# Rows of the sixth slot on turned by DMA instead of TensorE, in a routed expert kernel on one core

## The reference

```python
e_idx = np.argmax(x @ w_gate, axis=1)
...
for e in range(E):                       # E = 8, F = 1024, D = 512
    mask = e_idx == e
    h = np.maximum(x[mask] @ w1[e], 0.0)
    ye = h @ w2[e]
    out[mask] = gate_w[mask, None] * eom[mask, e, None] * ye
```

## Time and profile before

| | |
|---|---|
| median of 3 runs | 860.55 us (859.25 to 861.95) |
| the profiled execution | 863.49 us |
| its span in the trace | 861.7 us |
| TensorE busy | 827.6 us, 96% of the span |
| VectorE, ScalarE, GpSimd busy | 572.5, 383.6, 180.2 us |
| mean granted TensorE clock | 0.995 of full speed |

### The profile page before, as it was taken

One profiled execution on the slowest core, in us unless ns is written; L12 is line 12 of the kernel. 1 busy time (PEld: TensorE's weight loads), 2 busy tenths in 40 slices (PEclk: granted clock), 3 DMA queues, 4 the chain that ended last, 5 costly groups with the idle time before them and its releaser, 6 DMA issues.

```text
span 861.7 us, 19310 instructions
## 1 busy us (share of the span) xinstructions
PE 827.6 (96%) x7018; PEld 549.2 (64%) x7019; DVE 572.5 (66%) x1200; ACT 383.6 (45%) x798; POOL 180.2 (21%) x208
## 2 busy tenths in 40 slices
PE   7999999999999999999999999999899999999995
PEld 5888777876555555555455555556577767777773
DVE  4778788877887998998898898855532444222221
ACT  5766667776555555555555555523111111111110
POOL 4444376663000001001001001010121222111100
PEclk9999999999999999999999999999999999999998
DMA  7255565541483884875784875485253852656610
GB/s 223 98 178 180 166 205 181 177 136 61 172 286 132 267 257 173 267 258 172 256 256 183 256 256 183 162 300 193 92 182 139 313 197 76 238 201 219 233 70 14
DMA packets 76554, 163.83 MB, mean 190 GB/s; under 512 B 39574, under 2 KB 43926, under 8 KB 69840
## 3 DMA queue, kind: packets, MB, share of 16 engines
q1 hardware_dynamic: 70576, 146.20, 50.3%
q0 software_dynamic: 5760, 16.80, 5.7%
q10 hardware_dynamic: 160, 0.07, 0.0%
HBM read 109.44 MB, written 47.47 MB: 182 GB/s over the span
## 4 chain that ended last, share of the span: by engine, by line
PE 70%; DVE 12%; issue 6%; DMA 5%; ACT 3%; POOL 2%; another core or an unknown queue 1%; DVEq 0%; POOLq 0%; ACTq 0%; SPq 0%
PE ps L876 18%; PE ps L865 15%; PE ps L971 11%; PE ps L959 11%; DMA arena<-split 4%; PE ps L781 4%; PE ps L726 3%; PE ps L753 3%; ACT arena L1073 2%; DVE arena L1256 2%; DVE arena L1510 2%; POOL arena L555 1%; PE ps L740 1%; DVE yrow L1475 1%; DVE relu L1566 1%
## 5 line engine op out<-in xcount | busy, mean ns | idle before, releaser
L865 PE MATMUL ps<-arena,w_in_sb 128*128 128x384 f16 x1152 | 200.9, 326 | 0.0
L876 PE MATMUL ps<-w_out_sb,arena 128*128 128x512 f16 x576 | 171.2, 379 | 5.0 <-DVE stage L1571 4.9
L865 PEld LDWEIGHTS ps<-arena,w_in_sb 128*128 128x128 f16 x1152 | 112.3, 98 | 80.9
L959 PE MATMUL ps<-x_sb,arena 128*128 128x128 f16 x2112 | 121.7, 219 | 3.9 <-DMA arena<-split 3.0
L959 PEld LDWEIGHTS ps<-x_sb,arena 128*128 128x128 f16 x2112 | 119.3, 98 | 8.1 <-issue 4.9
L1233 ACT ACTIVATE x_sb<-ps 128x512 f16<-128x512 f32 x54 | 31.6, 596 | 206.7 <-PE ps L959 172.4
L971 PE MATMUL ps<-arena,x_sb 128*128 128x512 f16 x528 | 119.7, 383 | 2.2 <-DVE x_sb L1667 2.2
L876 PE MATMUL ps<-w_out_sb,stage 128*128 128x512 f16 x288 | 109.1, 379 | 0.0
L1073 ACT ACTIVATE arena<-ps,arena 128x128 f32<-128x128 f32 x288 | 79.4, 382 | 55.4 <-DVE arena L1258 51.2
L1205 ACT ACTIVATE arena<-relu 128x384 f16<-128x384 f32 x96 | 50.0, 521 | 109.5 <-DVE relu L1566 108.3
L876 PEld LDWEIGHTS ps<-w_out_sb,arena 128*128 128x128 f16 x576 | 55.8, 98 | 65.4 <-issue 7.2
(11 more groups left out here) (210 smaller groups left out, 976.9 us busy)
## 6 DMA issues: line engine op xcount, KB each, us to landing
arena<-split SPq DMA_DIRECT2D x36, 1024.0 KB
arena<-in_moe_w SPq DMA_DIRECT2D x16, 2048.0 KB
split<-arena SPq DMA_DIRECT2D x16, 2048.0 KB, 7.5
arena<-in_qkt SPq DMA_DIRECT2D x15, 576.0 KB, 6.2
stage<-in_moe_w_in SPq DMA_DIRECT2D x16, 512.0 KB, 4.1
stage<-in_moe_w_out SPq DMA_DIRECT2D x16, 512.0 KB, 5.3
x_sb<-rows POOLq DMA_DIRECT2D x27, 257.0 KB
arena<-in_v SPq DMA_DIRECT2D x32, 128.0 KB, 4.4
```

Source lines behind the costliest of these rows:

```text
L865: last = nc.tensor.matmul(ps[:, HB[f % GB], 0:BN], w_in_sb[:, lw, c, f * P:(f + 1) * P], xt[:, a, lx, c, :], start=c == 0 and lw + lx == 0 ...
L876: last = nc.tensor.matmul(ps[:, YB + r, :], g_sb[lg_][:, f % GB, r * P:(r + 1) * P], w_out_sb[:, lw, f, :], start=f == 0 and lg_ + lw == 0 ...
L959: last = nc.tensor.matmul(ps[:, bank, f % 4 * P:(f % 4 + 1) * P], w1_sb[b][:, lw, c, f * P:(f + 1) * P], xgt[:, a, lx, c, :], start=c == 0 ...
```

## The change

Rows of slots 0 to 4 are turned on TensorE as before. From slot 5 (`TURN_AT`) on, ScalarE issues one DMA transpose for a slot: it reads the slot's rows from `xg` and writes them turned into a new buffer `turned`; VectorE copies that into `xgt` in place of the PSUM bank. There are four row buffers (`XB4`) and four turned buffers. ScalarE issues the DMA for slot s + 4 right after the relus of slot s, and waits for the rows' load before it. GpSimd loads slot s + 5 right after it has stored slot s. The loops over slots of ScalarE, VectorE and GpSimd are written out; TensorE keeps its loop, without the transposes.

```diff
+XB4, TURN_AT = 4, 5
...
-        xg = spare[:, 0:2 * XW].rearrange("p (a d) -> p a d", a=2)
+        xg = spare[:, 0:XB4 * XW].rearrange("p (a d) -> p a d", a=XB4)
+        turned = spare[:, 14336:14336 + XB4 * 2 * DM].rearrange("p (a k n) -> p a k n", a=XB4, k=2 * DC)
...
@@ GpSimd
-            def next_load(s, a):
-                row = slot_start(s)
-                pool.wait_ge(xg_read, s - 1)
+            def load(s, row=None):
+                row = slot_start(s) if row is None else row
+                if s >= XB4:
+                    pool.wait_ge(xg_read, s - XB4 + 1)
                 carry()
-                load(row, a)
+                pool.dma_start(xg_words[:, s % XB4, :], rows[bass.ds(row, P), :]).then_inc(xg_loaded[s % XB4], 16)
...
-            for s in range(EARLY, EARLY + 2):
-                load(starts[s - EARLY], s % 2)
+            for s in range(EARLY, EARLY + 4):
+                load(s, starts[s - EARLY])
             store(1, 1, True)
-            for s in range(EARLY + 2, EARLY + 4):
-                next_load(s, s % 2)
-            store(2, 0, True)
-            next_load(7, 1)
-            store(3, 1, True)
-            with pool.Fori(0, (SLOTS - 9) // 2) as i:
-                for a in range(2):
-                    next_load(i * 2 + (a + 8), a)
-                    store(i * 2 + (a + 4), a)
-            next_load(SLOTS - 1, 0)
-            for s in range(SLOTS - 5, SLOTS):
-                store(s, s % 2)
+            for s in range(2, SLOTS):
+                store(s, s % 2, s < 4)
+                if s + 5 < SLOTS:
+                    load(s + 5)
@@ TensorE
             def used_slot(s, a, need, b):
                 slot_hidden(a, b)
-                if more:
-                    slot_transposes(s + 2, a, turn)
                 pe.wait_ge(ew2_loaded, need)
                 pe.wait_ge(og_ready, s - 1)
                 slot_output(s, a, b)
@@ ScalarE
+            def turn_rows(s):
+                a = s % XB4
+                act.wait_ge(xg_loaded[a], s // XB4 * 16 + 16)
+                if s >= TURN_AT + XB4:
+                    act.wait_ge(xgt_ready, s - XB4 + 1)
+                act.dma_start_transpose(turned[:, a], xg[:, a, 0:2 * DM]).then_inc(turned_rows[a], 16)
             relu_slot(1, 1)
             relu_slot(2, 0)
-            with act.Fori(0, (SLOTS - 3) // 2) as i:
-                relu_slot(i * 2 + 3, 1)
-                relu_slot(i * 2 + 4, 0)
+            for s in range(TURN_AT, TURN_AT + 2):
+                turn_rows(s)
+            for s in range(EARLY, SLOTS):
+                relu_slot(s, s % 2)
+                if s + 4 < SLOTS:
+                    turn_rows(s + 4)
@@ VectorE
             def slot_in(s, a, bank=None):
-                dve.wait_ge(xg_transposed, s + 1)
+                if s < TURN_AT:
+                    dve.wait_ge(xg_transposed, s + 1)
+                    src = ps[:, a if bank is None else bank, :].bitcast(F16)
+                else:
+                    dve.wait_ge(turned_rows[s % XB4], (s - TURN_AT) // XB4 * 16 + 16)
+                    src = turned[:, s % XB4].rearrange("p k n -> p (k n)")
```

More of the change, by code:

```diff
@@ L299, in moe_program @@
         table_ready = sem("table_ready")
-        xg_loaded = [sem(f"xg_loaded{a}") for a in range(2)]
+        xg_loaded = [sem(f"xg_loaded{a}") for a in range(XB4)]
+        turned_rows = [sem(f"turned_rows{a}") for a in range(XB4)]
         ew1_loaded = sem("ew1_loaded")
@@ L655, in _ @@
             pool.wait_ge(early_ready, 1)
-            starts = [slot_start(s) for s in range(2)]
+            starts = [slot_start(s) for s in range(EARLY)]
             pool.wait_ge(pads_stored, 16 * E)
             pool.wait_ge(scattered, 16 * BT * (BLOCKS - 1))
-            for s in range(2):
-                load(starts[s], s)
-            next_load(2, 0)
+            for s in range(EARLY):
+                load(s, starts[s])
             scatter(BLOCKS - 1)
@@ L941, in mlp_block, with slot_transposes @@
                         ranks(n - 1)
-            def slot_transposes(s, a, turn, bank=None):
-                bank = a if bank is None else bank
-                pe.wait_ge(xg_loaded[a], turn * 16)
+            def slot_transposes(s, bank):
+                a = s % XB4
+                pe.wait_ge(xg_loaded[a], s // XB4 * 16 + 16)
                 for l in range(2):
@@ L1008, in _, with used_slot @@
             slot_output(2, 0, 0, (0,))
-            slot_transposes(3, 1, 2)
+            slot_transposes(3, 1)
             slot_output(2, 0, 0, (1,))
-            slot_transposes(4, 0, 3)
-            def used_slot(s, a, turn, more, need, b):
+            slot_transposes(4, 0)
+            def used_slot(s, a, need, b):
                 slot_hidden(a, b)
-                if more:
-                    slot_transposes(s + 2, a, turn)
                 pe.wait_ge(ew2_loaded, need)
@@ L1019, in used_slot, with slot @@
                 slot_output(s, a, b)
-            def slot(s, a, turn, more=True):
+            def slot(s, a):
                 p = s - EARLY
@@ L1041, in _ @@
             with pe.Fori(0, (SLOTS - 5) // 2) as i:
[L1042 to L1045, removed]
+                slot(i * 2 + 3, 1)
+                slot(i * 2 + 4, 0)
+            slot(SLOTS - 2, 1)
+            slot(SLOTS - 1, 0)
         @block.scalar
@@ L1653, in slot_in @@
             def slot_in(s, a, bank=None):
-                bank = a if bank is None else bank
-                dve.wait_ge(xg_transposed, s + 1)
-                if not isinstance(s, int) or s > 1:
+                if s < TURN_AT:
[4 more added lines that the diff above has]
+                    src = turned[:, s % XB4].rearrange("p k n -> p (k n)")
+                if s > 1:
                     dve.wait_ge(eh_done, s * 2 - 2)
-                nc.vector.tensor_copy(xgt[:, a].rearrange("p l c n -> p (l c n)"), ps[:, bank, :].bitcast(F16)).then_inc(xgt_ready, 1)
-                nc.vector.tensor_tensor(slot_scale[:, bass.ds(s, 1)], xg_words[:, a, DM:DM + 1], slot_inv[:, bass.ds(s, 1)], ALU.mult)
-                nc.vector.tensor_copy(slot_token[:, bass.ds(s, 1)], xg_words[:, a, DM + 1:DM + 2].bitcast(I32)).then_inc(xg_read, 1)
+                nc.vector.tensor_copy(xgt[:, a].rearrange("p l c n -> p (l c n)"), src).then_inc(xgt_ready, 1)
+                words = xg_words[:, s % XB4]
+                nc.vector.tensor_tensor(slot_scale[:, s:s + 1], words[:, DM:DM + 1], slot_inv[:, s:s + 1], ALU.mult)
+                nc.vector.tensor_copy(slot_token[:, s:s + 1], words[:, DM + 1:DM + 2].bitcast(I32)).then_inc(xg_read, 1)
             def slot_lo(s, a, banks=None, halves=(0, 1)):
@@ L1761, in _ @@
             slot_in(4, 0)
[L1762 to L1766, removed]
+            for s in range(EARLY, SLOTS):
+                slot(s, s % 2, s // 2, s + 2 < SLOTS)
 def lay_out_heads(_np, q, k):
```

20 lines of the change are left out of this document (8 added, 12 removed).

## The result

The changed kernel takes 889.11 us (median of 4 runs, 888.52 to 893.38), the kernel before 861.09 us on the same chip (4 runs, 859.25 to 861.95): ratio 1.0341, 95% interval 1.0321 to 1.036, so 28.0 us slower. Forecast were 881 us and a range of 866 to 892.

The account below looks back on a forecast made before the run. The prediction took TensorE's own work to bound the kernel. Its terms, -9.9 - 2.3 + 8.4 + 15.4 + 8.5, summed to +20.1 us, set on the median of 860.55: 881 us, range 866 to 892.

Parts of the forecast that it names:

- The five waits: TensorE's w2 product waits behind five empty slots, since ScalarE's relu is queued behind a row-load wait: twice 6 to 10 us, three times about 3.
- 22 slots without transposes: Slots 5 to 26 lose their TensorE transposes, 0.45 us each, all on its path: 9.9 us less.
- old waits swallowed: Two earlier waits just behind empty slots, 0.87 and 1.4 us, vanish inside the new stalls: 2.3 us less.
- two long waits (slots 6, 8): At slots 6 and 8, beside weight loads, TensorE waits 7.7 us each, bounds 2.7 and 14: 15.4 us more.
- three short waits (10, 12, 14): At empty slots 10, 12 and 14 TensorE waits 2.8 us each for ScalarE: 8.4 us more.
- clock behind the five: All five stalls exceed 2.18 us, so TensorE's clock falls to 0.50: 1.7 us each, 8.5 in all, between 0 and about 12.
- VectorE's copy, the DMA engines' load: VectorE's copy from SBUF and 29 us of DMA transposes cost nothing; at worst 2.7 us beside slot 9's weight load.
- From trace to median: Profiled execution lay 2.9 us above the median of the runs, so the sum was set on 860.55 us, giving 880.7.
- ScalarE is not held: Rival: ScalarE is past the DMA issue by 4 us at empty slots; kernel gets faster, 852.0 us; chance 0.11.
- The clock stays: Rival: ScalarE is held, but TensorE's clock stays at 2.4 GHz behind the stalls, 872.2 us; chance 0.14.
- Rows land as if alone: Rival: row loads at slots 6 and 8 are not slowed, 2 x 5.0 us less, 870.7 us; chance 0.08.
- A longer issue: Rival: the DMA issue takes 3.05 us from ScalarE, 7.2 us more, 888 us; chance 0.10.

Follow-up runs that it names:

- light weights: Changed kernel with weight loads from the third expert on cut to 16 KB instead of 1 MB each: 875.28 us, ratio 1.0179.
- three ahead: Changed kernel with ScalarE issuing the DMA transpose for slot s + 3, not s + 4: 868.9 us, ratio 1.0089; with the weight loads cut, 852.46 us.
- the bare wait: Against the kernel transposing for slot s + 3, ScalarE also waits for the load of slot s + 4 after each issue: 891.42 us, ratio 1.0386.
- load ahead of the store: Changed kernel with GpSimd issuing the load of slot s + 5 before the store of slot s: 892.69 us, ratio 1.0404; weight loads cut, 852.48 us.
- the weights spaced out: SyncE issues transposes and weights, row load before store; fourth expert's weights moved from after slot 8 to after slot 11: 854.94 us, ratio 0.9937.

## Why the prediction was right, point by point

The five waits, their place and their cause were right. The time was 8 us short, 5.8 of it in the terms and 2.2 in the step from the trace to the median. Against the 25.8 us between the spans:

| term | predicted | measured |
|---|---|---|
| 22 slots without transposes | -9.9 | -9.9 |
| old waits swallowed | -2.3 | -2.0 (3.8 to 1.8 us) |
| two long waits (slots 6, 8) | +15.4 | +13.1 |
| three short waits (10, 12, 14) | +8.4 | +9.9 |
| clock behind the five | +8.5 | +13.3 |
| products behind the five no longer overlap the ones ahead | 0 | +0.8 |
| the loop over slots starts later | 0 | +0.7 |
| sum | +20.1 | +25.9 |

- **Transposes.** 40 matmuls are left, and a slot takes 10.54 us after the last empty one. Right.
- **VectorE's copy, the DMA engines' load.** Costed at nothing. In the changed kernel that held: the longest landing was 7.8 us, and no wait of TensorE stands for a turned row. It held, it seems, because ScalarE issues so late there that the transposes seldom meet the weights; the versions that issue earlier point that way. In the kernels that issue in time the same term was 2 to 5% of the whole. The prediction's bound for it, 2.7 us, was worked out from transposes issued by SyncE, and it would have misled anyone who took "free ScalarE" as the whole cure.
- **Short waits.** 3.3 us each and not 2.8. The row load took 2.91 to 3.25 us where 2.4 were taken from the earlier trace rows; the issue, 1.25 us, was as cheap as its least value.
- **Long waits.** 6.28 and 6.86 us and not 7.7. The row load landed 6.9 us after its issue, where 6.5 had been read from the earlier trace rows, but ScalarE's issue beside the weights took 1.29 and 1.25 us and not 2.0. The upper bound of 14 us does not follow from its terms: 681.0 + 7.44 + 1.35 - 676.7 is 13.1. The forecast does not use it. The two long waits came out 2.3 us too short and the three short ones 1.5 us too long, so these two errors hid each other in part.
- **The clock is the mis-sized term.** The prediction took 1.7 us for each wait from the one stretch of 2.18 us in the earlier trace rows, and put the end of the range for it at 12. The five w2 products took 7.51, 7.86, 8.10, 8.23 and 8.29 us in the timeline, where an undisturbed one takes 5.34: 2.2 to 3.0 each, 13.3 in all. (In the chain an undisturbed one counts 5.18, since 0.16 us of it overlaps the product ahead; behind a wait it does not, which is the 0.8 us of the table.) They start with the clock at 0.50 and stay there for most of their length. The Trainium skill, "TensorE: Matmul & The Clock Gate", section "HAM oscillation — how this bites in real kernels", describes the same pattern, in which each wait for data is paid a second time in products at the low clock; the trace agrees, and adds that the size is not fixed: the same kernel with light weights had waits of 2.6 to 3.5 us and paid 4.7 us in all. The prediction's step from "longer than 2.18 us" to "the clock falls" is not general either: behind waits of 2.62 and 3.47 us in that kernel it did not fall. That it fell at all five places here was in part luck.
- **From trace to median.** The sum was set on the median before, 860.55. The runs show 28.0 us between the medians and 25.8 between the profiled spans. The profiled execution of before lay 2.4 us above the median of its runs, the one of the changed kernel at its median. That is the remaining 2.2 us.
- **The rivals.** "ScalarE is not held" fell by the five waits. "The clock stays" fell by the windows at 0.50. "Rows land as if alone" fell by the landing of 6.9 us. "A longer issue" fell by 1.25 us.

The place of the cause was tested from both sides. Taking the wait out of ScalarE's way removed the five waits (three ahead). Putting the bare wait back restored them. And with the collision gone the wait is worth 22.8 us, twice over by two ways of removing it (852.46 and 852.48 us).

Open is why packets of a transpose, beside weights, can last 0.177 us instead of 0.019, while in another kernel they keep to 0.022. And the clock's price after a wait of 3.3 to 3.5 us was 0 to 3.0 us; what decides it was not found.

## What to carry to other kernels

A DMA issue was cheap here, 1.25 us at the median, though one took 14.3 us in a kernel crowded with transfers. The wait in front of it is another matter: it belongs to the engine that issues the DMA. Before a DMA is put into a compute engine's stream, look at what is queued behind it in the thinnest spot of the schedule, here an empty slot. Work moved from a bound engine to the DMA engines has to be costed against the transfers that it will meet once it is issued in time, not against those that it meets now. And price an idle stretch of TensorE with what it does to the products behind it; here that was 13 us on top of 23.

## What the runs showed of the hardware

- A DMA transpose of 256 KB (about 1,060 packets of 250 bytes) lands in 3.1 us alone. Beside weights from another queue it landed after up to 20.2 us (three ahead) and 30.8 us (load ahead of the store), and in the second over 12 us all transfers together fell to 65 GB/s.
- In one stream with the weights, issued behind an expert's last piece, the longest landing was 13.2 us, and 8.4 with the weights spaced out.
- ScalarE's issue of such a transpose is 1.25 us at its median and was 14.3 us once, in the kernel with the load ahead of the store, and TensorE waited 9.2 us for it.
- After idle stretches of 3.3 to 6.9 us TensorE's granted clock was 0.50 in the changed kernel, and 24 matmuls of 512 columns took 7.5 to 8.3 us instead of 5.34. In the same kernel with light weights the clock stayed at 1.00 after 2.62 and 3.47 us and fell after 3.29 to 3.38. Matmuls issued into the wait kept the product at 5.34 us.
- Longer or more TensorE loops came with more instruction packets, 39 with a body of four slots and 25 with four loops against 11, and with waits for "issue" of up to 5.6 and 5.8 us.
